# Attention and two feed-forward layers on one core: transposed tiles through four PSUM banks, and an extra copy on VectorE

## The chip, the cores and the metric

The kernel runs on one core of a Trainium2 chip. The metric is the time of one execution on the device in microseconds (us), the median over runs.

## What is computed

The reference first computes attention for 4 batches of 8 heads, 576 positions of 64 values: causal softmax attention, mixed by a gate for each head with a linear memory read.

```python
scores = scale * np.matmul(q, k.transpose(0, 1, 3, 2))
...
local = np.matmul(a, v)
...
q_p = phi(q)
mem_ret = np.einsum('bhsd,bhde->bhse', q_p, M_prev)
mem_norm = np.einsum('bhsd,bhd->bhs', q_p, z_prev)[..., None] + 1e-06
...
return (g * mem_out + (1 - g) * local).astype(np.float32)
```

The result, as 2304 tokens of 512 values, goes through two gated feed-forward layers (512 to 1536 and back, 512 to 2048 and back).

## The kernel before

**Two stages.** The attention stage takes the heads in 16 pairs (NPAIR), one pair after the other. The second stage, the two feed-forward layers, is a long run of matrix products for TensorE: up products (L1312 to L1314, from `product`) and down products. Sums that it needs of its weights and of the tokens are in part made by ScalarE, VectorE and GpSimd during the attention stage.

**A pair.** The 576 query rows of a head are one block of 64 and four blocks of 128. `tile_of(j)` gives the pair p and the tile i, and the tiles run from 4 down to 1 (tile i covers the keys up to its own block; tile 1 also has the first block of 64). For each tile TensorE computes the scores of both heads (`scores`, L1232, the first block in `scores_f`, L1242); VectorE adds the mask, negates, and takes the maxima (`tile_max`, L927); ScalarE takes the exponentials and their row sums into `rown` (`exp_tile`, L683 and L688); GpSimd puts the scaled memory rows beside them (`mem_rows`, L564), by a factor from VectorE's `mem_scale` (L946). TensorE then transposes `rown` in chunks of 128 columns (`turn`, L1261), into PSUM; a copy brings the transposed chunks into `pt` in SBUF (`copy_pt`, on ScalarE L704, on VectorE L965); and TensorE multiplies them with the values (`values`, L1287 and L1282).

**Groups and banks.** The chunks of a tile are turned in groups of two to four (GROUPS), nine groups for each pair. A group fills part of one PSUM bank, and one copy takes it out. Groups alternate between banks 4 and 5, in the order of their number n over the whole kernel, and before group n TensorE waits for the copy of group n-2. The copy of group (4, 1), the second of tile 4, is VectorE's (ON_DVE); the other eight are ScalarE's. Banks 0 to 3 hold scores. The value products go to bank 6 (tiles 4 and 3) and bank 7 (tiles 2 and 1).

**The way out.** VectorE computes the denominators and their reciprocals (`sums_inverse`, L953 and L956). TensorE transposes the reciprocals with the last group of the pair (L1265); ScalarE copies the row out (L702); SP writes it to memory in two transfers (L438, L439) and reads it back, broadcast, in two (L447). `out_x` on VectorE (L973) multiplies the value products in bank 6 (part 0) and bank 7 (part 1) with it and writes x. Each `out_x` raises `x_done`.

**TensorE's order in iteration p** is: scores of tile 4 of pair p; the last group of tile 4 and both groups of tiles 3, 2 and 1 of pair p-1, with the row-sum transpose at their end; the first-block scores of pair p; values of tile 4 of pair p-1; scores of tiles 3, 2 and 1 of pair p; the first two groups of tile 4 of pair p; values of tiles 3, 2 and 1 of pair p-1.

**VectorE's order in iteration p** is: mem_scale of tile 1 and sums_inverse of pair p-1; out_x part 0 of pair p-2; tile_max of tile 4 of pair p; out_x part 1; the norm sums (`norm_q`, `rnorm_q`); low parts for the next stage in some of the pairs (L982, L991); then mem_scale of tile 4, tile_max of tiles 3, 2 and 1, mem_scale of tile 3, the copy of group (4, 1), mem_scale of tile 2, and `phi` of the next pair (L901), from which GpSimd makes its products with z (`phi_z`, L545 and L547). All orders are written out by hand, and each engine works through its own in order.

Of the kernel before, what the change touches and what calls it, by code (L numbers as in the profile page):

```python
# [11 lines left out]
P = 128  # L12


def attention_two_ffns(nc, qk_in, nat_in, vm_in, beta, w_up, w_down, out):

    NPAIR = qk_in.shape[0]
# [6 lines left out]
    NBLK = 2 * NT - 1  # L24
# [45 lines left out]
    with ctx:  # L70
# [244 lines left out]
        def tile_of(j):  # L315

            return j // SLOTS, SLOTS - j % SLOTS
# [9 lines left out]


        GROUPS = {4: ((0, 4), (4, 8), (8, 10)), 3: ((0, 4), (4, 8)), 2: ((0, 3), (3, 6)), 1: ((0, 3), (3, 5))}
        ON_DVE = ((4, 1),)  # L330
        PER_PAIR = sum(len(g) for g in GROUPS.values())
        DVE_PER_PAIR = len(ON_DVE)
        ACT_PER_PAIR = PER_PAIR - DVE_PER_PAIR
# [1 line left out]
        def groups_before(j):  # L335

            return PER_PAIR * (j // SLOTS) + sum(len(GROUPS[SLOTS - k]) for k in range(j % SLOTS))

        def group_at(n):

            j = SLOTS * (n // PER_PAIR)
            n -= groups_before(j)
            while n >= len(GROUPS[tile_of(j)[1]]):
                n -= len(GROUPS[tile_of(j)[1]])
                j += 1
            return j, n
# [7 lines left out]
        def copied(j, g):  # L354

            d = dve_copies(j, g)
            if (tile_of(j)[1], g) in ON_DVE:
                return pt_dve, d + 1
            return pt_act, groups_before(j) + g - d + 1

        def group_bank(j, g):

            return 4 + (groups_before(j) + g) % 2

        def chunk_col(i, n):

# [24 lines left out]

        def ends_pair(j, g):

            return tile_of(j)[1] == 1 and g == 1

        def r_rows(j):

            return ps[0:NBLK, group_bank(j, 1), 2 * P:3 * P]


        def out_place(i):
# [265 lines left out]
        def _(act):  # L667
# [7 lines left out]
            def exp_tile(j):  # L675

                p, i = tile_of(j)
                w = width(i)
                at_least(act, turned, groups_before(j - ROWN + 1) if j >= ROWN else 0)
                for h in range(2):  # L680
                    t, k = 2 * j + h, block_of(i, h)
                    at_least(act, maxed, t + 1)
                    nc.scalar.activation(head_rows(j)[:, h + (i == 1), D:D + w], negs[:, t % NEGS, 0:w], ACT.Exp,  # L683
                                         bias=nmax[:, p % 2, k:k + 1], scale=-1.0,
                                         accum_out=rsum[:, p % 2, k:k + 1]).then_inc(expd, 1)
                if i == 1:
                    at_least(act, maxedf, p + 1)
                    nc.scalar.activation(head_rows(j)[:, 0, D:2 * D], negf[:, p % 2], ACT.Exp,  # L688
                                         bias=nmax[:, p % 2, 0:1], scale=-1.0,
                                         accum_out=rsum[:, p % 2, 0:1]).then_inc(expdf, 1)  # L690

            def copy_pt(j, gs):

                at_least(act, pv_done, j - PTS + 1)
                for g in range(len(GROUPS[tile_of(j)[1]])):
                    if g not in gs or (tile_of(j)[1], g) in ON_DVE:
                        continue
                    at_least(act, turned, groups_before(j) + g + 1)
                    if ends_pair(j, g):
                        p = tile_of(j)[0]  # L700
                        at_least(act, r_out, 32 * (p - 1))
                        nc.scalar.activation(rrow[0:NBLK, p % 2], r_rows(j), ACT.Copy).then_inc(r_row, 1)  # L702
                    dst, src = group_ends(j, g)
                    nc.scalar.activation(dst, src, ACT.Copy).then_inc(pt_act, 1)  # L704
# [35 lines left out]
            for p in range(NPAIR + 1):  # L740
                j = SLOTS * p
                if p > 0:
                    copy_pt(j - SLOTS, (2,))
                    for k in range(1, SLOTS):
                        copy_pt(j - SLOTS + k, (0, 1))
                if p < NPAIR:
                    exp_tile(j)
                if p + 1 < NPAIR:
                    exp_q(p + 1)
                if p < NPAIR:  # L750
                    exp_tile(j + 1)
                    copy_pt(j, (0, 1))
                    exp_tile(j + 2)
                    exp_tile(j + 3)
                for m, u, n in HIGH_AT:
                    if m == p:
                        up_high(u, n)
                for m, n in X_HIGH_AT:
                    if m == p:
                        x_high(0, n)  # L760
# [132 lines left out]
        def _(dve):  # L893
# [74 lines left out]
            def out_x(p, part):  # L968

                at_least(dve, pv_done, SLOTS * p + (2 if part == 0 else SLOTS))  # L970
                at_least(dve, r_in[p % 2], 32 * (p // 2 + 1))
                dst, o, r = x_part(p, part)
                nc.vector.tensor_tensor(dst, o, r, ALU.mult).then_inc(x_done, 1)  # L973
# [41 lines left out]
            phi(0)  # L1015
            for p in range(NPAIR + 2):
                j = SLOTS * p
                if 0 < p <= NPAIR:
                    mem_scale(j - 1)
                    sums_inverse(p - 1)  # L1020
                if p > 1:
                    out_x(p - 2, 0)
                if 0 < p < NPAIR:
                    tile_max(j)
                if p > 1:
                    out_x(p - 2, 1)
                if p < NPAIR:
                    norm_q(p)
                    dve.wait_ge(gt_set, 3)
                    rnorm_q(p)  # L1030
                for m, u, n in HIGH_AT:
                    if m == p - 1 and n > 0:
                        up_low(u, n)
                for m, n in X_HIGH_AT:
                    if m == p - 1:
                        x_low(0, n)
                if p < NPAIR:
                    mem_scale(j)
                    for k in range(1, SLOTS):
                        tile_max(j + k)  # L1040
                    mem_scale(j + 1)
                    copy_pt(j)
                    mem_scale(j + 2)
                if p + 1 < NPAIR:
                    phi(p + 1)
# [164 lines left out]
        def _(pe):  # L1210
# [34 lines left out]
            def turn(j, gs):  # L1245

                p, i = tile_of(j)
                at_least(pe, expd, 2 * (j + 1))
                at_least(pe, memd, j + 1)
                if i == 1:  # L1250
                    at_least(pe, expdf, p + 1)
                for g in range(len(GROUPS[i])):
                    if g not in gs:
                        continue
                    n = groups_before(j) + g
                    if n >= 2:
                        pe.wait_ge(*copied(*group_at(n - 2)))
                    a, b = GROUPS[i][g]
                    for c in range(a, b):
                        col = chunk_col(i, c)  # L1260
                        mm = nc.tensor.transpose(ps[:, group_bank(j, g), (c - a) * P:(c - a + 1) * P],  # L1261
                                                 rown[:, j % ROWN, col:col + P], ident[:])
                    if ends_pair(j, g):
                        pe.wait_ge(rdend, p + 1)
                        mm = nc.tensor.transpose(r_rows(j), rden[:, p % 2], ident[:])  # L1265
                    mm.then_inc(turned, 1)

            def values(j):

                p, i = tile_of(j)  # L1270
                s = p % 2
                bank, col = out_place(i)
                if i == 4:
                    at_least(pe, v_scaled, p + 1)
                    at_least(pe, x_done, 2 * p - 1)
                if i == 2:
                    at_least(pe, x_done, 2 * p)
                for g in range(len(GROUPS[i])):
                    pe.wait_ge(*copied(j, g))
                if i == 1:  # L1280
                    for h in range(2):
                        nc.tensor.matmul(ps[D * h:D * h + D, bank, 0:D], vm[:, s, h, 0], pt[:, j % PTS, 0, D * h:D * h + D],  # L1282
                                         start=True, stop=True)
                for c in range(i + 1):
                    for h in range(2):
                        n = (i + 1) * h + c + (i == 1)
                        mm = nc.tensor.matmul(ps[D * h:D * h + D, bank, col:col + P], vm[:, s, h, c],  # L1287
                                              pt[:, j % PTS, n], start=(c == 0), stop=(c == i))
                mm.then_inc(pv_done, 1)
# [147 lines left out]
```

## Time and profile before

| | |
|---|---|
| median of 3 runs | 1016.28 us (1015.73 to 1016.39) |
| the profiled execution | 1015.94 us |
| its span in the trace | 1014.1 us |
| busy, share of the span | TensorE 97%, VectorE 79%, ScalarE 57%, GpSimd 49% |
| attention stage | to about 199.7 us, when the first up product starts |

The span runs from the first to the last instruction. "Idle before" an instruction is followed by what ended it. The engines are named PE (TensorE), PEld (its weight loads), DVE (VectorE), ACT (ScalarE), POOL (GpSimd) and SP.

### The profile page before, as it was taken

What the parts mean: (1) busy time and instruction counts of PE and PEld (TensorE: products, weight loads), DVE (VectorE), ACT (ScalarE), POOL (GpSimd) and SP (SyncE); (2) the same over time, 40 slices, a digit from 0 to 9 for tenths busy, and PEclk for the clock granted to TensorE, in tenths of its full rate; (3) what the DMA queues carried; (4) which work ended last, traced back from release to release, by engine and by line L of the source; (5) the groups of instructions that cost most, each with busy time, mean ns of one, the idle gap of its engine ahead of it and who ended that gap; (6) DMA issues with size and microseconds to landing.
All of it is one profiled execution on the core that took longest, in us unless ns stands there. A gap on an engine that the chain in (4) does not pass through costs nothing.

```text
span 1014.1 us, 19135 instructions
## 1 busy us (share of the span) xinstructions
PE 982.9 (97%) x6328; PEld 919.6 (91%) x6328; DVE 799.9 (79%) x1422; ACT 573.1 (57%) x1130; POOL 501.5 (49%) x407
## 2 busy tenths in 40 slices
PE   6999999999999999999999999999999999999998
PEld 4777777788999999999999998999989999899997
DVE  5778888556788776778767789888897888988776
ACT  5898898755445544446444445545554546555451
POOL 5666766256675432454333476575543435432330
PEclk9999999999999999999999999999999999999999
DMA  6454443134334333233333323324132522225211
GB/s 228 145 155 161 155 143 118 50 125 146 104 111 144 114 112 104 104 106 125 105 104 107 124 82 104 116 72 146 63 125 65 185 101 87 97 91 187 68 37 63
DMA packets 34782, 116.13 MB, mean 115 GB/s; under 512 B 4224, under 2 KB 4608, under 8 KB 34688
## 3 DMA queue, kind: packets, MB, share of 16 engines
q1 hardware_dynamic: 34544, 114.91, 33.9%
q8 instruction: 55, 0.90, 0.4%
q14 instruction: 39, 0.32, 0.1%
q10 hardware_dynamic: 144, 0.00, 0.0%
HBM read 100.14 MB, written 14.75 MB: 113 GB/s over the span
## 4 chain that ended last, share of the span: by engine, by line
PE 85%; DVE 5%; issue 4%; ACT 4%; POOL 1%; DMA 1%; DVEq 0%; ACTq 0%; POOLq 0%
PE ps L1312 24%; PE ps L1313 23%; PE ps L1314 23%; PE ps L1261 5%; PE ps L1287 5%; PE ps L1232 5%; ACT pt L704 2%; DVE xt_l L991 1%; DVE xy L1106 1%; DVE hid_l L1084 1%; DVE hid_r L1096 1%; ACT rown L683 1%; DMA qk<-qk_in 0%; ACT tmp L806 0%; DVE hb L1061 0%
## 5 line engine op out<-in xcount | busy, mean ns | idle before, releaser
L589 POOL TENSOR_TENSOR wu_l<-wu_r,wu_h 128x768 fp32r<-128x768 f32 (+1 forms) x75 | 142.1, 1902 | 399.0 <-ACT wu_h L713 399.0
L1312 PE MATMUL ps<-xt_h,wu_h 128*128 128x384 f32 x840 | 283.2, 337 | 5.5 <-DVE xt_l L991 2.8
L1314 PE MATMUL ps<-xt_h,wu_l 128*128 128x384 f32 x840 | 280.9, 334 | 0.0
L1313 PE MATMUL ps<-xt_l,wu_h 128*128 128x384 f32 x840 | 280.9, 334 | 0.0
L1312 PE MATMUL ps<-hid_h,wd_h 128*128 128x384 f32 x672 | 226.4, 337 | 6.3 <-DVE xy L1106 5.6
L1314 PE MATMUL ps<-hid_h,wd_l 128*128 128x384 f32 x672 | 224.7, 334 | 0.0
L1313 PE MATMUL ps<-hid_l,wd_h 128*128 128x384 f32 x672 | 224.7, 334 | 0.0
L1106 DVE TENSOR_TENSOR xy<-xy,ps 128x384 f32<-128x384 f32 x288 | 157.1, 548 | 48.4 <-PE ps L1314 47.4
L791 ACT ACTIVATE hid_h<-hid_r 128x768 fp32r<-128x768 f32 x84 | 70.8, 842 | 198.7 <-DVE hid_r L1080 141.9
L1312 PEld LDWEIGHTS ps<-xt_h,wu_h 128*128 128x128 f32 x840 | 157.6, 188 | 13.7 <-issue 11.8
L1313 PEld LDWEIGHTS ps<-xt_l,wu_h 128*128 128x128 f32 x840 | 157.7, 188 | 0.0
L1314 PEld LDWEIGHTS ps<-xt_h,wu_l 128*128 128x128 f32 x840 | 157.7, 188 | 0.0
L595 POOL TENSOR_TENSOR wd_l<-wd_r,wd_h 128x512 fp32r<-128x512 f32 x84 | 136.1, 1633 | 15.0 <-ACT wd_h L718 13.9
L1312 PEld LDWEIGHTS ps<-hid_h,wd_h 128*128 128x128 f32 x672 | 126.1, 188 | 12.4 <-issue 8.0
L982 DVE TENSOR_TENSOR wu_l<-wu_r,wu_h 128x512 fp32r<-128x512 f32 x105 | 123.8, 1179 | 8.0 <-DMA kept<-wu_r 3.9
L1313 PEld LDWEIGHTS ps<-hid_l,wd_h 128*128 128x128 f32 x672 | 126.2, 188 | 0.0
L1314 PEld LDWEIGHTS ps<-hid_h,wd_l 128*128 128x128 f32 x672 | 126.1, 188 | 0.0
L713 ACT ACTIVATE wu_h<-wu_r 128x512 fp32r<-128x512 f32 (+1 forms) x180 | 118.9, 694 | 0.0
L1084 DVE TENSOR_TENSOR hid_l<-hid_r,hid_h 128x768 fp32r<-128x768 f32 x84 | 85.8, 1022 | 36.9 <-ACT hid_h L791 36.8
L683 ACT ACTIVATE rown<-negs,nmax 128x576 f32<-128x576 f32 (+3 forms) x128 | 77.0, 603 | 12.3 <-DVE nmax L927 12.3
L1261 PE MATMUL ps<-ident,rown 128*128 128x128 f32 x464 | 74.2, 286 | 7.8 <-ACT pt L704 2.5
L1261 PEld LDWEIGHTS ps<-ident,rown 128*128 128x128 f32 x464 | 49.4, 142 | 30.0 <-ACT pt L704 16.1
(84 smaller groups left out, 1319.3 us busy)
## 6 DMA issues: line engine op xcount, KB each, us to landing
wu_r<-w_up SPq DMA_DIRECT2D x60, 512.0 KB, 4.7
wd_r<-w_down SPq DMA_DIRECT2D x42, 512.0 KB, 3.7
wu_r<-kept SPq DMA_DIRECT2D x38, 512.0 KB, 5.5
kept<-wu_r SPq DMA_DIRECT2D x19, 512.0 KB, 4.5
qk<-qk_in SPq DMA_DIRECT2D x15, 640.0 KB, 5.1
nat<-nat_in SPq DMA_DIRECT2D x16, 384.0 KB, 3.1
vm<-vm_in SPq DMA_DIRECT2D x16, 320.0 KB, 3.6
rbc<-rsums SPq DMA_DIRECT2D x32, 144.0 KB, 3.1
```

The costliest lines, as they stand in the source:

```text
L589: nc.gpsimd.tensor_tensor(wu_l[u % 3][:, a:b], wu_r[u % 3][:, a:b], wu_h[u % 2][:, a - 1:b - 1].bitcast(F32), ALU.subtract).then_inc(low_p ...
L595: nc.gpsimd.tensor_tensor(wd_l[:, t % 6], wd_r[:, t % 6], wd_h[:, t % 6].bitcast(F32), ALU.subtract).then_inc(wd_lo, 1)
L683: nc.scalar.activation(head_rows(j)[:, h + (i == 1), D:D + w], negs[:, t % NEGS, 0:w], ACT.Exp, bias=nmax[:, p % 2, k:k + 1], scale=-1.0, ...
L713: nc.scalar.activation(wu_h[u % 2][:, a - 1:b - 1], wu_r[u % 3][:, a:b], ACT.Copy).then_inc(wu_hi[n], 1)
L791: nc.scalar.activation(hid_h[:, t % 6], hid_r[:, t % 6], ACT.Copy).then_inc(hh_done, 1)
L982: nc.vector.tensor_tensor(wu_l[u % 3][:, a:b], wu_r[u % 3][:, a:b], wu_h[u % 2][:, a - 1:b - 1].bitcast(F32), ALU.subtract).then_inc(low_d ...
L1084: nc.vector.tensor_tensor(hid_l[:, t % 6], hid_r[:, t % 6], hid_h[:, t % 6].bitcast(F32), ALU.subtract).then_inc(hl_done, 1)
L1106: nc.vector.tensor_tensor(y, y, o, ALU.add).then_inc(evac, 1)
L1261: mm = nc.tensor.transpose(ps[:, group_bank(j, g), (c - a) * P:(c - a + 1) * P], rown[:, j % ROWN, col:col + P], ident[:])
L1312: nc.tensor.matmul(dst, w_hi, v_hi, start=start, stop=False, skip_group_check=onto)
L1313: nc.tensor.matmul(dst, w_hi, v_lo, start=False, stop=False, skip_group_check=onto)
L1314: return nc.tensor.matmul(dst, w_lo, v_hi, start=False, stop=stop, skip_group_check=onto)
```

## The change

Each group gets a fixed bank from a table, among four banks: (4,0), (4,2), (2,1) and (1,1) use bank 4; (4,1), (3,0) and (1,0) bank 5; (3,1) bank 6; (2,0) bank 7. `group_under` finds the group that used the same bank last, and the turn waits for its copy. Before a turn into bank 6 or 7 TensorE also waits for the x multiplication of that bank of the pair before, and the values of tile 4 wait for the copy of (3,1). The row-sum transpose moves from the last group of the pair to the one before it. On VectorE both out_x move to the head of the iteration, and a copy, that of group (2,0), is added behind tile_max of tile 4. On ScalarE the exponentials of tile 2 move ahead of the copy of (4,0).

```diff
--- before.py
+++ after.py
@@ -327,7 +327,11 @@
 
         GROUPS = {4: ((0, 4), (4, 8), (8, 10)), 3: ((0, 4), (4, 8)), 2: ((0, 3), (3, 6)), 1: ((0, 3), (3, 5))}
-        ON_DVE = ((4, 1),)
+        ON_DVE = ((4, 1), (2, 0))
+
+
+
+        BANK = {(4, 0): 4, (4, 1): 5, (4, 2): 4, (3, 0): 5, (3, 1): 6, (2, 0): 7, (2, 1): 4, (1, 0): 5, (1, 1): 4}
         PER_PAIR = sum(len(g) for g in GROUPS.values())
         DVE_PER_PAIR = len(ON_DVE)
         ACT_PER_PAIR = PER_PAIR - DVE_PER_PAIR
@@ -360,7 +364,15 @@
 
         def group_bank(j, g):
 
-            return 4 + (groups_before(j) + g) % 2
+            return BANK[tile_of(j)[1], g]
+
+
+        def group_under(j, g):
+
+            n = groups_before(j) + g - 1
+            while n >= 0 and group_bank(*group_at(n)) != group_bank(j, g):
+                n -= 1
+            return group_at(n) if n >= 0 else None
 
         def chunk_col(i, n):
 
@@ -391,11 +403,11 @@
 
         def ends_pair(j, g):
 
-            return tile_of(j)[1] == 1 and g == 1
+            return tile_of(j)[1] == 1 and g == 0
 
         def r_rows(j):
 
-            return ps[0:NBLK, group_bank(j, 1), 2 * P:3 * P]
+            return ps[0:NBLK, group_bank(j, 0), 3 * P:4 * P]
 
         def out_place(i):
@@ -749,8 +761,8 @@
                     exp_q(p + 1)
                 if p < NPAIR:
                     exp_tile(j + 1)
+                    exp_tile(j + 2)
                     copy_pt(j, (0, 1))
-                    exp_tile(j + 2)
                     exp_tile(j + 3)
                 for m, u, n in HIGH_AT:
                     if m == p:
@@ -1015,15 +1027,16 @@
             phi(0)
             for p in range(NPAIR + 2):
                 j = SLOTS * p
+                if p > 1:
+                    out_x(p - 2, 0)
+                    out_x(p - 2, 1)
                 if 0 < p <= NPAIR:
                     mem_scale(j - 1)
                     sums_inverse(p - 1)
-                if p > 1:
-                    out_x(p - 2, 0)
                 if 0 < p < NPAIR:
                     tile_max(j)
-                if p > 1:
-                    out_x(p - 2, 1)
+                if 0 < p <= NPAIR:
+                    copy_pt(j - 2)
                 if p < NPAIR:
                     norm_q(p)
                     dve.wait_ge(gt_set, 3)
@@ -1252,9 +1265,10 @@
                 for g in range(len(GROUPS[i])):
                     if g not in gs:
                         continue
-                    n = groups_before(j) + g
-                    if n >= 2:
-                        pe.wait_ge(*copied(*group_at(n - 2)))
+                    if group_under(j, g):
+                        pe.wait_ge(*copied(*group_under(j, g)))
+                    if group_bank(j, g) >= 6:
+                        at_least(pe, x_done, 2 * (p - 1) + group_bank(j, g) - 5)
                     a, b = GROUPS[i][g]
                     for c in range(a, b):
                         col = chunk_col(i, c)
@@ -1273,6 +1287,7 @@
                 if i == 4:
                     at_least(pe, v_scaled, p + 1)
                     at_least(pe, x_done, 2 * p - 1)
+                    pe.wait_ge(*copied(j + 1, 1))
                 if i == 2:
                     at_least(pe, x_done, 2 * p)
                 for g in range(len(GROUPS[i])):
```

## Rows read from the trace of the kernel before

**Rows 1.** Busy time of each engine over the span, from the page.

```profile
PE 982.9 (97%) x6328; PEld 919.6 (91%) x6328; DVE 799.9 (79%) x1422; ACT 573.1 (57%) x1130; POOL 501.5 (49%) x407
```

**Rows 2.** Row-sum transposes: count, duration min/median/max in ns, first and last start.

```profile
L1265 PE MATMUL ps<-ident,rden x16: 272/273/273, 21.4 to 196.1; 128*9 128x128 f32 x16
```

**Rows 3.** Stretches: length; PE, PEld, DVE, ACT, POOL busy (count); granted clock, DMA, GB/s.

```profile
145.00:156.63 11.63, 11.27 (x114) 8.30 (x115) 9.92 (x33) 10.55 (x31) 7.99 (x10) 1.00 0.48 150
199.60:211.20 11.60, 11.60 (x70) 11.54 (x67) 4.41 (x10) 5.59 (x9) 0.00 (x0) 1.00 0.47 129
```

**Rows 4.** Timeline of TensorE's weight loads: start, length, count, idle before.

```profile
87.94 0.64 PEld L1261 LDWEIGHTS ps<-ident,rown 128*128 128x128 f32 x6
88.92 0.42 PEld L1261 LDWEIGHTS ps<-ident,rown 128*128 128x128 f32 x4 [0.34 <-ACT pt L704]
...
90.88 0.31 PEld L1261 LDWEIGHTS ps<-ident,rown 128*128 128x128 f32 x3 [0.31 <-issue]
91.39 0.20 PEld L1261 LDWEIGHTS ps<-ident,rown 128*128 128x128 f32 x2 [0.20 <-ACT pt L704]
...
91.67 0.30 PEld L1242 LDWEIGHTS ps<-qk 128*128 128x128 f32 x2
...
95.10 0.86 PEld L1261 LDWEIGHTS ps<-ident,rown 128*128 128x128 f32 x8 [0.23 <-issue]
```

**Rows 5.** Timeline of ScalarE in the same pair.

```profile
88.48 0.38 ACT L704 ACTIVATE pt<-ps 128x256 f32<-128x256 f32 x1
88.92 0.60 ACT L704 ACTIVATE pt<-ps 128x512 f32<-128x512 f32 x1
...
90.27 0.49 ACT L704 ACTIVATE pt<-ps 128x384 f32<-128x384 f32 x1
...
91.98 0.27 ACT L702 ACTIVATE rrow<-ps 9x128 f32<-9x128 f32 x1
92.15 0.36 ACT L704 ACTIVATE pt<-ps 128x256 f32<-128x256 f32 x1
92.41 0.76 ACT L683 ACTIVATE rown<-negs,nmax 128x576 f32<-128x576 f32 x1
...
95.08 0.67 ACT L683 ACTIVATE rown<-negs,nmax 128x448 f32<-128x448 f32 x1 [0.48 <-DVE nmax L927]
```

**Rows 6.** Timeline of VectorE in the same pair.

```profile
87.73 0.16 DVE L946 SCALAR_TENSOR_TENSOR mscale<-rsum,rnorm 128x3 f32<-128x3 f32 x1 [0.40 <-ACT rown L688]
...
89.30 0.37 DVE L973 TENSOR_TENSOR xy<-ps,rbc 128x256 f32<-128x256 f32 x1
89.59 0.75 DVE L927 CUSTOM_DVE_ANT_0 negs<-ps,mask 128x576 f32<-128x576 f32 x1
...
90.94 0.49 DVE L973 TENSOR_TENSOR xy<-ps,rbc 128x320 f32<-128x320 f32 x1
...
97.04 0.68 DVE L965 COPY pt<-ps 128x512 f32<-128x512 f32 x1
98.09 0.16 DVE L946 SCALAR_TENSOR_TENSOR mscale<-rsum,rnorm 128x2 f32<-128x2 f32 x1 [0.37 <-ACT rown L683]
```

**Rows 7.** Timeline of SP's transfers in the same pair.

```profile
92.99 0.62 SPq L439 DMA_DIRECT2D rsums<-rrow  x1
94.77 1.13 SPq L447 DMA_DIRECT2D rbc<-rsums  x2
```

**Rows 8.** The 32 reads of the row sums, L447.

```profile
DMA to landing us min/median/max: 2.8/3.1/4.6
```

**Rows 9.** Timeline of GpSimd in the same pair.

```profile
87.83 1.27 POOL L547 TENSOR_TENSOR qz<-qp,nat 128x512 f32<-128x512 f32 x1
...
94.36 0.40 POOL L564 TENSOR_TENSOR rown<-qp,mscale 128x128 f32<-128x128 f32 x1 [1.97 <-DVE mscale L946]
```

**Rows 10.** The 16 denominators, L953: durations in ns.

```profile
L953 DVE TENSOR_SCALAR den<-rsum x16: 172/1292/1297, 18.6 to 192.5; 128x9 f32<-128x9 f32 x16
```

**Rows 11.** VectorE's copies from PSUM in the later stage, L1103.

```profile
L1103 DVE COPY xy<-ps x48: 543/552/559, 238.0 to 916.1; 128x384 f32<-128x384 f32 x48
```

## The prediction, made before the changed kernel ran

> **What bounds the kernel now.** The page first: TensorE is busy 97% of the span [rows 1], at the full granted clock in the stretches looked at [rows 3]. So only time in which TensorE stands still, or its instruction count, can move the end. The change touches nothing behind the attention stage, so the second view is that stage's own beat. The transpose of the reciprocal row sums comes once for each of the 16 pairs, first at 21.4 us and last at 196.1 us [rows 2]: 174.7 / 15 = 11.65 us for each pair. The up products behind the stage leave TensorE no pause (11.60 of 11.60 us busy), so what the stage gives back reaches the end; within a pair ScalarE is busy 10.55 of 11.63 us and VectorE 9.92 [rows 3].
>
> The third view is TensorE's weight loads in one pair, because every transpose begins with one and the idle time stands before it. The section with the last group of tile 4 and all of tiles 3, 2 and 1 begins at 87.94 and ends with the load for the first-block scores at 91.67: 3.73 us for 21 transposes and that of the row sums. Eight transposes without a pause take 0.86 us, 0.108 each, so 22 would take 2.38. The missing 1.35 us is in five gaps of 0.20 to 0.34, one ahead of each group from the third on (three of them shown) [rows 4]. ScalarE's copies show why: with two banks, group n waits for the copy of group n-2. Tile 4's last copy ends at 88.48 + 0.38 = 88.86 and the next group starts at 88.92; the copy of (2,0) ends at 90.76 and (1,0) starts at 90.88 [rows 4, 5]. Outside this section TensorE has no pause in the pair that waits for another engine. So the loop is: turn, copy, turn, five times, and then TensorE's own work.
>
> **What the four banks take away.** Group (3,1) goes to bank 6 and (2,0) to bank 7, where their last users are the two x products. Then the first five groups need only the copies of (4,2), done at 88.86, and (3,0). Run through from 87.94 at 0.108: (3,0) at 88.22, (3,1) at 88.66, (2,0) at 89.09, (2,1) at 89.42 (bank 4, free since 88.86), (1,0) at 89.75 (bank 5, freed by the copy of (3,0) at 88.92 + 0.60 = 89.52). The row-sum transpose follows at 90.07; it is only moved, at no cost in itself. (1,1) could start at 90.18, but shares bank 4 with (2,1).
>
> ScalarE by then: back to back, a copy starts 0.09 before the one before it ends (91.98 with 0.27 is followed at 92.15, that with 0.36 at 92.41) [rows 5]. (3,0) 88.92 to 89.52, (3,1) 89.43 to 90.03; (2,0) is VectorE's now; (2,1) 89.94 to 90.43. TensorE follows 0.05 later, at 90.48. So one wait of 0.30 us is left of five. Before, (1,1) started at 91.39 and the first-block scores 0.28 behind it; the row-sum transpose, 0.11 of that, is now in front, so 0.17 is left: 90.48 + 0.17 = 90.65 against 91.67. **Gain 1.02 us for each section.**
>
> **What the added wait costs.** (3,1) and (2,0) now wait for the two x multiplications of the pair before, and behind them in TensorE's queue stands everything. They used to start at 89.30 and 90.94 [rows 6]; at those places they would stop TensorE for 0.3 and then nearly 2 us. They are moved to the head of VectorE's order, behind phi, where VectorE was idle 0.40 us before 87.73. At 0.29 and 0.40 start to start they end near 88.1: ahead of 88.66 and 89.09. The values they read were all produced by 86.8. They also need the broadcast row sums: the second write is issued at 92.99, the reads from 94.77 on, in 1.13 for the two [rows 7], and a read landed in 3.1 in the median and 4.6 at worst [rows 8]. One period back the second of them is there at 86.8, in the median, against 87.33, where phi ends. The row is copied 1.5 us earlier in the new order (ScalarE reaches it at 90.4, not 91.98), in a period that is 1.0 shorter: the slack grows by 0.5. I take nothing for this wait. SP's reads of the row sums, and what waits for x before the sums of the next stage, get x earlier than before; the order of SP and GpSimd is not touched. The value product of tile 4, in bank 6 too, now waits for the copy of (3,1), which ends at 90.03, before the product's turn.
>
> **What is queued behind the moved work.** The mem_scale of tile 1 goes from 87.73 [rows 6] to about 88.1. GpSimd, its reader, comes to it only at 89.1, after the product with z that starts at 87.83 and takes 1.27 [rows 9]: covered. If GpSimd were ahead, (1,0) would be late by up to 0.4, of which 0.30 is under the remaining copy wait. The denominator is stretched anyway: 1.29 us in the median, 0.17 at the least, in the last section, where GpSimd had no such product to do [rows 10]; here it ends with GpSimd's product. So a later start leaves its end, and the maxima of the next tile 4 start at 89.30 in place of 89.59; at 1.35 for both [rows 6] their last result is there at 90.73, just as the first-block scores need it. Here the margin is about nothing.
>
> The Trainium skill, SBUF — State Buffer, section "SBUF: two separate sides", says the pair of ports that VectorE and GpSimd share is an exclusive lock, held for a whole instruction; the two lengths of the denominator agree. It speaks against the change in one point: mem_scale has two SBUF inputs and would now fall inside GpSimd's product and be held to its end (rival 1). By it the sum would be 1.02 - 0.29 a section; by the rows alone, 1.02.
>
> **The extra copy on VectorE.** The trace has no 128x384 copy to pt on VectorE; the same shape from PSUM takes 0.55 in the later stage [rows 11], between a bound of 0.68 (the 128x512 copy at 97.04) [rows 6] and nothing if it falls into idle time. I take 0.55, 0.47 start to start. It stands behind the maxima, so at 90.65 to 91.2; its reader, the value product of tile 2, runs more than 3 us later. On VectorE it delays the norm sums, but those start at 91.12 and not 91.34, as two x multiplications have left. ScalarE loses 0.40 start to start: before (1,1), and so tile 4's exponentials start at 91.3 and not 92.41. What hangs on them is GpSimd's memory rows, which ended at 94.36 + 0.40 = 94.76 [rows 9]; now 1.1 earlier, 93.7, for the next turn of tile 4 at 95.10 - 1.02 = 94.08 [rows 4]: covered by 0.4.
>
> **Two exponentials ahead of tile 4's first copy.** ScalarE idles 0.48 before the exponentials of tile 3 at 95.08 [rows 5], and tile 2's maxima are there by the time it ends these. The copy moves back by two 128x320 exponentials, 1.09 us; it then ends near 97.0, and its bank is next written at the following section's start, at 98.5. Nothing on either side.
>
> **Sum.** 16 sections: 16 x 1.02 = 16.3 us. The profiled execution took 1015.94, 0.34 below the median of 1016.28; the difference is taken from the median: **1000.0**. Bounds: with no wait left, 16 x 1.35 = 21.6, 994.7.
>
> **Rivals.**
> 1. VectorE late for the first-block scores. mem_scale is held until 89.1, the denominator comes after it, the maxima end 0.29 later: 16 x 0.73 = 11.7, 1004.6. For it: the margin of nothing. Against: tile 2's exponentials now come before the copy, so phi and GpSimd's product start earlier in the pair by some 0.4. 14%.
> 2. VectorE becomes the bound. 9.92 busy in a pair with a low part of x [rows 3], plus 0.47, plus its short pauses and the 0.37 it waited for tile 2's exponentials before 98.09 [rows 6]: 11.1 at worst, 16 x 0.53 = 8.5, 1007.8. Against: 1.1 of the 9.92 is the denominator's waiting, which shrinks as the queue gets later. 12%.
> 3. Slower: the row sums' round trip becomes a loop. Row-sum transpose, copy (0.36), two writes (0.75), 1.78 until the reads, 0.53, landing 3.1 to 3.4, x multiplications 0.8, (2,0) to the row-sum transpose 1.3: 8.9 us in the median, 10.4 with a landing of 4.6. It decides from 11.6 on, that is 2.7 us more in the two transfers than in the median. At 12.0 it gives +16 x 0.4 = +6.4, 1022.7. 8%. Between 10.6 and 11.6 it eats the gain.
> 4. The change does not show: the next stage waits for the last x anyway, or the loop of 3 stands at today's beat: 1016. Against: no pause in the 11.6 us of up products, with the last x product inside them [rows 3]. 6%.
> 5. The last wait vanishes too: 994.7. 6%.
>
> **Chances.** The forecast, 998 to 1002, 54%; rivals 14, 12, 8, 6, 6. A measurement of this kernel tells 0.2%, 2 us. Faster 54 + 14 + 12 + 6 = 86%, same 6%, slower 8%. The range takes the forecast, rivals 1 and 2 and the edge of 5: 995 to 1008.5; alone, the forecast has 998 to 1002.
>
> **What would show it.** Row-sum transposes 10.6 us apart; in each section one idle gap of the weight loads, 0.3 us, ahead of the last group, and none before (3,1) or (2,0); the x multiplications ending before 88.66 of this pair's clock; denominator stretched to GpSimd's end still; VectorE with a 128x384 copy of 0.55. Wrong if a gap before (3,1) is ended by VectorE's x product or by the row-sum DMA (rival 3), if one stands before the first-block scores, ended by the maxima (rival 1), or if ScalarE's exponentials of tile 4 come late for its turn.

## The result, and the profile after

The changed kernel takes 1000.34 us in the median of four runs (999.02 to 1001.57), the kernel before 1016.17 in four (1015.73 to 1016.39). The ratio is 0.9845, with a 95% interval of 0.9827 to 0.9862: 15.8 us less. The forecast was 1000.0. The profiled execution took 999.02, the lowest of the four; its span is 997.2. Below, "stage" is the time up to the first up product of the profiled execution: 199.66 before, 184.86 after, 14.80 less.

From the page after, the busy time of each engine over the span:

```profile
PE 970.6 (97%) x6328; PEld 920.4 (92%) x6328; DVE 795.7 (80%) x1438; ACT 562.7 (56%) x1114; POOL 503.8 (51%) x407
```

The 16 copies have gone from ScalarE (1130 to 1114) to VectorE (1422 to 1438); TensorE has the same 6328 instructions in 16.9 us less span. VectorE's busy time does not rise with the 16 copies (8.8 us): summed over the trace its mem_scales take 8.4 us more and its denominators 17.0 us less. The 4.2 us by which it falls lie in other groups, mostly low parts for the second stage (L982, now L994, 2.4 less), and no run was made for them. Here are these groups. First the row-sum transposes, then the denominators and the mem_scales (count, duration in ns, first and last start):

```profile
L1279 PE MATMUL ps<-ident,rden x16: 272/273/273, 20.7 to 180.8; 128*9 128x128 f32 x16
...
L965 DVE TENSOR_SCALAR den<-rsum x16: 157/159/174, 19.5 to 179.0; 128x9 f32<-128x9 f32 x16
...
L958 DVE SCALAR_TENSOR_TENSOR mscale<-rsum,rnorm x64: 150/158/962, 13.6 to 178.9; 128x2 f32<-128x2 f32 x48, 128x3 f32<-128x3 f32 x16
```

The beat is (180.8 - 20.7) / 15 = 10.67 us against 11.65 [rows 2]. No denominator is stretched any more, where 1292 ns was the median [rows 10]; mem_scales of up to 962 ns have come instead. One pair in the middle, with a low part of x (columns as in [rows 3]):

```profile
133.80:144.49 10.69, 10.49 (x118) 8.33 (x113) 9.88 (x34) 9.85 (x29) 7.96 (x9) 1.00 0.51 158
```

TensorE has the full clock here too. VectorE and ScalarE are both within 0.85 us of the beat now. Next one pair's weight loads, as in [rows 4]:

```profile
82.75 2.05 PEld L1275 LDWEIGHTS ps<-ident,rown 128*128 128x128 f32 x19
84.77 0.09 PEld L1279 LDWEIGHTS ps<-ident,rden 128*9 128x9 f32 x1
85.35 0.20 PEld L1275 LDWEIGHTS ps<-ident,rown 128*128 128x128 f32 x2 [0.49 <-ACT pt L716]
85.52 0.30 PEld L1255 LDWEIGHTS ps<-qk 128*128 128x128 f32 x2
85.89 1.07 PEld L1302 LDWEIGHTS ps<-pt,vm 128*64 128x64 f32 x20
```

The turning section (the last group of tile 4 and all groups of tiles 3, 2 and 1, up to the load for the first-block scores) runs from 82.75 to 85.52, 2.77 us against 3.73, with 19 transposes in one piece and one gap, ahead of (1,1). The view counts 0.49 from the end of the last load; from the row-sum load (84.77) to the next is 0.58 where 0.11 is the pace, so some 0.47 is lost there. ScalarE and VectorE in the same pair:

```profile
83.28 0.39 ACT L716 ACTIVATE pt<-ps 128x256 f32<-128x256 f32 x1
...
83.72 1.09 ACT L716 ACTIVATE pt<-ps 128x512 f32<-128x512 f32 x2
...
84.81 0.49 ACT L716 ACTIVATE pt<-ps 128x384 f32<-128x384 f32 x1
```

```profile
81.57 0.81 DVE L985 TENSOR_TENSOR xy<-ps,rbc 128x256 f32<-128x256 f32 x2
82.53 0.93 DVE L958 SCALAR_TENSOR_TENSOR mscale<-rsum,rnorm 128x3 f32<-128x3 f32 x1
83.38 0.16 DVE L965 TENSOR_SCALAR den<-rsum 128x9 f32<-128x9 f32 x1
...
84.37 0.75 DVE L939 CUSTOM_DVE_ANT_0 negs<-ps,mask 128x576 f32<-128x576 f32 x1
...
85.05 0.55 DVE L977 COPY pt<-ps 128x384 f32<-128x384 f32 x1
```

The x multiplications end at 82.38, before the section begins, so (3,1) and (2,0) never wait for them. The maxima end at 85.12, 2.37 after the section's start. GpSimd beside it:

```profile
82.15 1.28 POOL L559 TENSOR_TENSOR qz<-qp,nat 128x512 f32<-128x512 f32 x1
```

mem_scale, 0.15 to 0.16 at the other tiles, is 0.93 long and ends at 83.46, with GpSimd's product (82.15 + 1.28 = 83.43). So it is in the other pairs: in this execution 14 of the 16 mem_scales of tile 1 start inside the product, take 0.20 to 0.96, and every one of them ends 0.02 to 0.03 behind it. The Trainium skill, SBUF — State Buffer, section "SBUF: two separate sides", has the ports that VectorE and GpSimd share as an exclusive lock, held for the whole instruction. The trace agrees: each mem_scale ends when the product does, whenever it started.

In the waits between 20 and 170 us (total us, times, longest), the two that decide between the forecast and rival 3:

```profile
PEld ps L1275 <- ACT pt L716: 6.4, 13, 0.5
...
DVE xy L985 <- DMA rbc<-rsums: 3.5, 5, 1.1
```

By the weight loads the one gap, 0.47 us, stands in every pair from the second to the fifteenth (13 of them in this window); VectorE waits for the row sums 5 times, 1.1 us at most, and TensorE never for x.

### The profile page after: what moved, and what is told of

The parts are those of the page before. It is cut to its first block, busy times and chain, and to the rows that moved or that the text cites. A ratio compares the mean times of both kernels' runs of the same rounds, so it can differ in the third digit from the quotient of the medians.

```text
span 997.2 us, 19181 instructions
## 1 busy us (share of the span) xinstructions
PE 970.6 (97%) x6328; PEld 920.4 (92%) x6328; DVE 795.7 (80%) x1438; ACT 562.7 (56%) x1114; POOL 503.8 (51%) x407
## 4 chain that ended last, share of the span: by engine, by line
PE 83%; DVE 6%; ACT 5%; issue 4%; DMA 1%; POOL 1%; SPq 0%; DVEq 0%; ACTq 0%; POOLq 0%
PE ps L1327 24%; PE ps L1329 23%; PE ps L1328 23%; PE ps L1302 5%; PE ps L1245 4%; ACT pt L716 3%; PE ps L1275 3%; DVE xt_l L1003 1%; DVE xy L1119 1%; DVE hid_l L1097 1%; DVE hid_r L1109 1%; ACT rown L695 1%; DMA qk<-qk_in 1%; DMA rbc<-rsums 0%; DVE negs L939 0%
## 5 line engine op out<-in xcount | busy, mean ns | idle before, releaser
L994 DVE TENSOR_TENSOR wu_l<-wu_r,wu_h 128x512 fp32r<-128x512 f32 x105 | 121.4, 1156 | 6.9 <-DMA kept<-wu_r 3.9
L818 ACT ACTIVATE tmp<-hb,nhalf 128x768 f32<-128x768 f32 x48 | 45.1, 940 | 50.8 <-issue 45.9
L1103 DVE SCALAR_TENSOR_TENSOR tmp<-tmp 128x768 f32<-128x768 f32 x48 | 54.9, 1144 | 19.3 <-ACT tmp L818 18.7
```

The source lines that it names most:

```text
L994: nc.vector.tensor_tensor(wu_l[u % 3][:, a:b], wu_r[u % 3][:, a:b], wu_h[u % 2][:, a - 1:b - 1].bitcast(F32), ALU.subtract).then_inc(low_d ...
L1103: nc.vector.scalar_tensor_tensor(tmp[:, r], tmp[:, r], 1.0, tmp[:, r], ALU.min, ALU.mult).then_inc(s_done, 1)
```

## The experiments

All are edits of the changed kernel. The beat is worked out from the first and last row-sum transpose, as above.

| kernel | median us | ratio to before, 95% | beat us | stage us |
|---|---|---|---|---|
| changed | 1000.34 | 0.9827 to 0.9862 | 10.67 | 184.86 |
| e5 two banks | 1014.62 | 0.9976 to 0.9995 | 11.53 | 198.16 |
| e1 copy on ScalarE | 1003.65 | 0.9866 to 0.9895 | 10.93 | 188.96 |
| e6 copy twice | 1000.60 | 0.9832 to 0.9861 | 10.67 | 184.58 |
| e2 copy before exponentials | 1002.61 | 0.9856 to 0.9885 | 10.86 | 187.70 |
| e3 row sums last | 1002.31 | 0.9849 to 0.9878 | 10.82 | 186.78 |
| e4 x late | 1034.32 | 1.0160 to 1.0194 | 12.98 | 220.5 |
| e7 last group later | 1001.92 | 0.9847 to 0.9877 | 10.83 | 187.01 |
| e8 GpSimd's order | 1025.07 | 1.0077 to 1.0111 | 12.33 | 208.9 |
| e9 with SP's order | 1000.38 | 0.9829 to 0.9856 | 10.71 | 184.46 |
| e10 last group in bank 6 | 998.24 | 0.9809 to 0.9836 | 10.62 | 183.54 |
| e11 e10 and e9 | 997.64 | 0.9806 to 0.9833 | 10.58 | 182.54 |

**The banks.** e5 keeps every order of the change, but takes two banks in turn and leaves the copy of (2,0) to ScalarE.

```
-            return BANK[tile_of(j)[1], g]
+            return 4 + (groups_before(j) + g) % 2
```

> All orders of the changed kernel (x first, row sums with the last group but one, tile 2's exponentials ahead of the copy), but banks 4 and 5 in turn as before, and all copies but (4,1) on ScalarE. Theory (the banks and the shorter chain of copies bring the gain): the gaps ahead of (3,1), (2,0), (2,1), (1,0) and (1,1) are all back, the beat is 11.5 to 11.65 us, 1013.5 to 1016.5 us. Rival (the orders bring it): 1000 to 1005.

1014.62, as expected: of the 15.8 us the orders alone give 1.3 (by the ratio, 0.5 to 2.4). So nearly all of the gain needs the banks. e1, next, differs from e5 only in the banks and their waits, and takes 1003.65: the banks give 11.0 us, and the copy's move to VectorE, on top of them, 3.3.

**The copy on VectorE.** e1 puts (2,0) back on ScalarE; e6 makes VectorE's copy of (2,0) twice, the second behind the first's end.

```
-        ON_DVE = ((4, 1), (2, 0))
+        ON_DVE = ((4, 1),)
```

> The changed kernel with the copy of group (2,0) back on ScalarE; banks, order and the rest as changed. Theory (the one wait left in a turning section stands on ScalarE's chain of copies up to that of (2,1)): the chain gets one 128x384 copy longer, 0.40 to 0.49 us, so the idle gap ahead of (1,1) grows from 0.37 to about 0.8 and the beat from 10.69 to about 11.1 us; 15 sections give +6 to +7, 1006 to 1008 us. Rival (the copy only balances work, the banks do it all): 1000 to 1001.

1003.65, 2.4 to 4.4 us less than expected. The weight loads show where, and why not more:

```profile
84.18 2.05 PEld L1275 LDWEIGHTS ps<-ident,rown 128*128 128x128 f32 x19
...
87.06 0.20 PEld L1275 LDWEIGHTS ps<-ident,rown 128*128 128x128 f32 x2 [0.76 <-ACT pt L716]
```

The gap ahead of (1,1) is 0.76, not 0.49: one more copy ahead of (2,1)'s costs 0.27 a section. In this pair it takes 0.37 start to start (86.13 to 86.50), and 0.10 of that falls into time in which ScalarE had been waiting for the turn of (2,1).

```
+                        if i == 2:
+                            nc.vector.tensor_copy(dst, src).then_inc(pt_more, 1)
+                            dve.wait_ge(pt_more, tile_of(j)[0] + 1)
                         nc.vector.tensor_copy(dst, src).then_inc(pt_dve, 1)
```

> The changed kernel with VectorE's copy of group (2,0) made twice, the second behind a wait for the first. Theory (VectorE has room behind the maxima of tile 4: it idles 0.97 us before mem_scale of tile 4): nothing, 999.5 to 1001.5 us, the idle time shrinks by about 0.6. Rival (VectorE is the bound or near it): +0.6 us a pair, 1006 to 1009.

1000.60 and an unchanged beat, as expected: VectorE has room for a second 0.55 us behind the maxima. It isn't the bound (rival 2).

**The exponentials first.** e2 puts tile 4's first copies back between the exponentials.

```
-                    exp_tile(j + 2)
                     copy_pt(j, (0, 1))
+                    exp_tile(j + 2)
```

> The changed kernel with ScalarE's order of before: the copy of (4,0) ahead of the exponentials of tile 2. Theory: bank 4 is due only in the next section, and the other side has slack too, so nothing or up to +0.1 us a section: 1000.3 to 1002 us, with mem_scale of tile 2, phi and GpSimd's product 0.4 us later in the beat. Rival (the maxima of tile 4 then come too late for the first-block scores): +0.3 us a section, 1004 to 1006.

1002.61; the beat is 0.19 longer, more than expected, though less than the rival's price. VectorE's order and TensorE's weight loads in one pair, one view after the other:

```profile
83.85 1.14 DVE L958 SCALAR_TENSOR_TENSOR mscale<-rsum,rnorm 128x3 f32<-128x3 f32 x1
84.92 0.16 DVE L965 TENSOR_SCALAR den<-rsum 128x9 f32<-128x9 f32 x1
...
85.91 0.75 DVE L939 CUSTOM_DVE_ANT_0 negs<-ps,mask 128x576 f32<-128x576 f32 x1
```

```profile
83.81 1.73 PEld L1275 LDWEIGHTS ps<-ident,rown 128*128 128x128 f32 x16
85.71 0.31 PEld L1275 LDWEIGHTS ps<-ident,rown 128*128 128x128 f32 x3 [0.17 <-issue]
...
86.42 0.20 PEld L1275 LDWEIGHTS ps<-ident,rown 128*128 128x128 f32 x2 [0.34 <-ACT pt L716]
86.79 0.30 PEld L1255 LDWEIGHTS ps<-qk 128*128 128x128 f32 x2 [0.17 <-issue]
```

Without the move, phi and GpSimd's product come later in the pair. mem_scale is held for 1.14, tile 1's memory rows are late for (1,0) (GpSimd ends them at 85.65; gap of 0.17), and the maxima end at 86.66, 2.85 after the section's start and not 2.37, so that the first-block scores wait as well. That is rival 1's mechanism; the swap on ScalarE is what keeps it off.

**The row sums' place.** e3 puts their transpose back behind (1,1).

```
-            return tile_of(j)[1] == 1 and g == 0
+            return tile_of(j)[1] == 1 and g == 1
```

> The changed kernel with the row-sum transpose back at the last group, (1,1). Theory: the transpose, 0.11 us, no longer lies in front of the copy wait but behind it, and the row of sums leaves about 0.5 us later, which the slack of its round trip takes: +0.11 us a section, 1001 to 1003 us, beat 10.8, and VectorE's idle time before the x multiplications, ended by the row-sum transfer, grows by about 0.4 us a pair. Rival (the round trip is already the loop that sets the beat): +0.5 us a section, 1007 or more.

1002.31, beat 0.15 longer, stage 1.92 longer. The transpose and its load fill 0.11 of the wait when they stand ahead of (1,1); that is 16 x 0.11 = 1.8. The other half of the expectation did not come: VectorE's idle time ended by the row-sum transfer is 3.0 us in 4 times between 20 and 170 us, not longer than the 3.5 of the changed kernel.

**x late.** e4 keeps the banks, but leaves the x multiplications where they were on VectorE.

```
+                if p > 1:
+                    out_x(p - 2, 0)
                 if 0 < p < NPAIR:
                     tile_max(j)
+                if p > 1:
+                    out_x(p - 2, 1)
```

> The changed kernel with the two x multiplications at their old places in VectorE's order, part 0 ahead of and part 1 behind the maxima of tile 4. Theory (the wait for x is free only because x leaves first): (3,1) waits for part 0, about 0.6 us, and (2,0) for part 1, until the maxima are done, so a section gets about 2.1 us longer than with the change: a beat of about 12.8 us, slower than the kernel before, 1028 to 1035 us. Rival (the row sums' round trip or the port lock sets the place of x anyway): under 1005.

1034.32, slower than before. In its waits between 20 and 170 us:

```profile
PE ps L1276 <- DVE xy L985: 18.2, 21, 1.1
```

Two of the four banks are x's; without x first TensorE waits for x 21 times, and the change costs 18 us instead of giving 16.

**Where the last wait can go.** e7 turns (1,1) after the values of tile 4, and copies it behind the exponentials of tile 4.

```
-                        copy_pt(j - SLOTS + k, (0, 1))
+                        copy_pt(j - SLOTS + k, (0, 1) if k < SLOTS - 1 else (0,))
...
-                        turn(SLOTS * (p - 1) + k, (0, 1))
+                        turn(SLOTS * (p - 1) + k, (0, 1) if k < SLOTS - 1 else (0,))
...
+                    turn(SLOTS * (p - 1) + SLOTS - 1, (1,))
```

> The changed kernel with the turn of the last group, (1,1), moved behind the values of tile 4 on TensorE, and its copy behind the exponentials of tile 4 on ScalarE. Theory (the wait ahead of (1,1), 0.37 us and 0.06 of restart, is the one left): it goes, but the first-block scores now wait for the maxima of tile 4, which end 2.38 us after the section's start against 2.24 for TensorE: about -0.23 us a section, beat 10.45, 996 to 998 us. Rival (GpSimd's scaling of the values, done 2.57 us after the section's start, or the exponentials of tile 4 take the wait's place): 1000 or more.

1001.92: a miss, and of the wrong sign.

```profile
105.45 2.06 PEld L1277 LDWEIGHTS ps<-ident,rown 128*128 128x128 f32 x19
...
107.95 0.30 PEld L1257 LDWEIGHTS ps<-qk 128*128 128x128 f32 x2 [0.38 <-issue]
108.35 1.10 PEld L1304 LDWEIGHTS ps<-pt,vm 128*64 128x64 f32 x20
109.63 0.20 PEld L1277 LDWEIGHTS ps<-ident,rown 128*128 128x128 f32 x2 [0.17 <-issue]
```

```profile
107.07 0.75 DVE L941 CUSTOM_DVE_ANT_0 negs<-ps,mask 128x576 f32<-128x576 f32 x1
```

The gap went to the first-block scores, 0.38, which now wait for the maxima (the last ends at 107.82, in the second view); they start at 2.50 after the section's start and not at 2.77. The 0.27 saved is what the two moved transposes take, and they come again behind, 0.20 long and with 0.17 of idle time on their way in. The expectation has no term for these 0.37.

e10 leaves the order and puts (1,1) in bank 6 instead, with the value products of tiles 4 and 3 in bank 7.

```
-        BANK = {(4, 0): 4, ..., (1, 0): 5, (1, 1): 4}
+        BANK = {(4, 0): 4, ..., (1, 0): 5, (1, 1): 6}
-            return (6, P * (i - 3)) if i >= 3 else (7, D + P * (i - 1))
+            return (7, P * (i - 3)) if i >= 3 else (6, D + P * (i - 1))
```

> The changed kernel with the last group, (1,1), in bank 6 in place of bank 4, and the value products of tiles 4 and 3 in bank 7, those of tiles 2 and 1 in bank 6; values of tile 4 wait for the copy of (2,0) in place of that of (3,1). Theory (the one wait left in a section is that of (1,1) for the copy of (2,1)): bank 6 is free 2.06 us after the section's start, TensorE comes at 2.24, so the gap of 0.49 goes; the first-block scores then follow the maxima, 2.44, and the values of tile 4 the copy of (2,0) at 2.85 to 2.9 in place of 3.14: beat 10.42 to 10.5, 996 to 997.5 us. Rival (VectorE's maxima and its copy take the whole wait over): 999.5 or more.

998.24: lower by 2.1 in the medians and 1.3 in the stage, less than expected. The intervals of the two kernels overlap, their runs do not (997.73 to 998.83 against 999.02 to 1001.57).

```profile
93.33 2.06 PEld L1275 LDWEIGHTS ps<-ident,rown 128*128 128x128 f32 x19
...
95.47 0.25 PEld L1275 LDWEIGHTS ps<-ident,rown 128*128 128x128 f32 x2
95.83 0.30 PEld L1255 LDWEIGHTS ps<-qk 128*128 128x128 f32 x2
96.36 1.10 PEld L1303 LDWEIGHTS ps<-pt,vm 128*64 128x64 f32 x20 [0.23 <-issue]
```

The wait ahead of (1,1) is gone. But the values of tile 4 start at 3.03 after the section's start, where the changed kernel has 3.14: they write bank 7 now and wait for VectorE's copy of (2,0), which stands behind the maxima and ends at 96.18 (95.63 + 0.55).

**What holds mem_scale.** e8 lets GpSimd make the product with z after tile 1's memory rows and the scaling of the values; e9 also moves SP's load for it behind the reads of the row sums. In e9:

```
-                if p + 2 < NPAIR:
-                    load_nat(p + 2)
                 if p > 1:
...
                 read_r(p - 1)
+                if p + 2 < NPAIR:
+                    load_nat(p + 2)
...
                     v_scale(p - 1)
+                    if p < NPAIR:
+                        phi_z(p)
```

> The changed kernel with GpSimd's products with z behind its memory rows of tile 1 and its scaling of the values, in place of ahead of them. Theory (mem_scale of tile 1 is held 0.93 us only because GpSimd's product is under way, and nothing but the first section pays for it): mem_scale back to 0.16 and the denominator at 0.16, the maxima of tile 4 earlier by about 0.7 us, the beat unchanged at 10.69, the first turning section shorter by about 0.8 us: 999 to 1000 us. Rival (the long mem_scale is not a held port but its own cost at that place): it stays at 0.9 and the time at 1000.3 or more.

1025.07, slower than before by 0.8 to 1.1%, where 999 to 1000 was expected: a miss, and of the wrong sign. mem_scale and denominator take 0.15 and 0.16, as expected (one mem_scale of tile 1 takes 0.39, inside GpSimd's memory rows), so it is what GpSimd does at the time that stretches them, and not their place on VectorE. The waits from 30 to 200 us and SP's transfers in one pair show what I had left out:

```profile
DVE xy L985 <- DMA rbc<-rsums: 29.7, 13, 3.7
```

```profile
110.09 0.33 SPq L439 DMA_DIRECT2D nat<-nat_in  x1
...
110.95 0.68 SPq L450 DMA_DIRECT2D rsums<-rrow  x1
...
114.30 1.12 SPq L459 DMA_DIRECT2D rbc<-rsums  x2
```

load_nat waits for the product (it overwrites its input), and the row sums' writes and reads stand behind it in SP's queue. Later product, later row sums, later x, and with x in front of everything on VectorE the banks come late (TensorE waits for x 11 times, 11.6 us together, in the same stretch): the loop of rival 3, with a beat of 12.33. It decides once something delays the row sums.

> The order of GpSimd of the run before (products with z behind the memory rows and the value scaling), and on SP the load of q rows for the pair after next moved behind the writes and reads of the row sums. Theory (the run before was slow because that load waits for the products with z, and the row sums queue behind it on SP): the row sums leave in time again, mem_scale takes 0.16, the maxima of tile 4 end 0.7 us earlier, the beat is that of the changed kernel, 10.69, as TensorE's turn of (2,1) and its copy set it; only the first section gains, 0.8 us: 998.5 to 1000.5 us. Rival (moving GpSimd's products costs by itself, through the norm sums and tile 4's memory rows): over 1003.

1000.38: with the load out of the way the 25 us are back, and the time is that of the changed kernel. So the held mem_scale costs nothing in the steady beat (10.71 by the table, 10.69 from section to section in most pairs of both kernels). It does in the first pair, whose rows are these: VectorE's and GpSimd's in the changed kernel, TensorE's there, TensorE's in e9.

```profile
18.65 0.96 DVE L958 SCALAR_TENSOR_TENSOR mscale<-rsum,rnorm 128x3 f32<-128x3 f32 x1 [0.83 <-ACT rown L695]
```

```profile
18.32 1.27 POOL L559 TENSOR_TENSOR qz<-qp,nat 128x512 f32<-128x512 f32 x1
```

```profile
17.78 1.74 PEld L1275 LDWEIGHTS ps<-ident,rown 128*128 128x128 f32 x16
20.27 0.31 PEld L1275 LDWEIGHTS ps<-ident,rown 128*128 128x128 f32 x3 [0.75 <-issue]
...
21.41 0.30 PEld L1255 LDWEIGHTS ps<-qk 128*128 128x128 f32 x2 [0.50 <-issue]
```

```profile
17.58 2.06 PEld L1275 LDWEIGHTS ps<-ident,rown 128*128 128x128 f32 x19
...
20.45 0.30 PEld L1255 LDWEIGHTS ps<-qk 128*128 128x128 f32 x2
```

There the first section takes 3.63 (17.78 to 21.41) in the changed kernel and 2.87 in e9. Of these 0.76 us the stage keeps 0.40 (184.46 against 184.86), and the medians show none.

**Both.** e11 is e10 with e9's edits.

> The two runs before together. Theory (without the last copy wait the section is held by VectorE's maxima and copy, which are late only because mem_scale of tile 1 is held by GpSimd's product): both waits go, TensorE runs through the section, beat 10.3 to 10.4, 994.5 to 996.5 us. Rival (the row sums' round trip, or tile 4's exponentials, now sets the beat): 997 or more.

997.64, the lowest of all, though not apart from e10 by the intervals. 994.5 to 996.5 was expected; the rival, that tile 4's exponentials or the row sums now set the beat, had 997 or more. In the pair below the section has no gap left; the next turn of tile 4 has one instead, 0.47 where the changed kernel has 0.23, right behind GpSimd's memory rows of tile 4 (97.57 + 0.40 = 97.97, second view):

```profile
92.01 2.06 PEld L1275 LDWEIGHTS ps<-ident,rown 128*128 128x128 f32 x19
...
94.36 0.30 PEld L1255 LDWEIGHTS ps<-qk 128*128 128x128 f32 x2
...
98.04 0.86 PEld L1275 LDWEIGHTS ps<-ident,rown 128*128 128x128 f32 x8 [0.47 <-issue]
```

```profile
97.57 0.40 POOL L576 TENSOR_TENSOR rown<-qp,mscale 128x128 f32<-128x128 f32 x1 [0.51 <-DVE mscale L958]
```

The product with z comes later, VectorE's norm sums wait for it (17.2 us in 15 times between 20 and 170), and tile 4's mem_scale and memory rows, which need the norms, are late. So it is neither of the rival's two, but the norms that come late.

## Why the prediction was right, and which terms were off

The time was right by the mechanism forecast: e5 and e1 show that the banks give it, e4 that it hangs on x first. That it was right to 0.3 us is luck: the stage gave 1.5 us less than the sum, about 1.0 came from where the sum had nothing, and the reason given for one term did not hold. The terms in turn:

- **Gain 1.02 us for each section.** 0.96 in the pair shown, and 11.65 - 10.67 = 0.98 of the mean beat. The forecast had the load of (1,1) 2.54 after the section's start; it came at 2.60. The gap is 0.47 and not 0.30, as TensorE also came to it 0.11 sooner than forecast (2.13, not 2.24), which costs nothing. The copy of (2,1) starts at 2.06, not 2.00: (3,0) and (3,1) were copied on time, but the copy of (2,1) could not start before its own turn was over, at 84.71. I had run ScalarE's chain back to back and not laid it against the turn.
- **Sum.** 16 sections were to give 16.3; the stage gave 14.80. The sum took one pair's section for all 16. By the weight loads of every pair, the thirteen sections like it went from 3.72 to 2.77, 0.07 short of the forecast each. The second (4.03 to 2.77) and the last (4.92 to 3.68) gave more, 1.26 and 1.24. The first gave only 0.33. These rows bound it in the kernel before:

```profile
17.60 0.64 PEld L1261 LDWEIGHTS ps<-ident,rown 128*128 128x128 f32 x6
...
21.56 0.30 PEld L1242 LDWEIGHTS ps<-qk 128*128 128x128 f32 x2
```

That is 3.96 against 3.63 after, with (1,0) waiting for memory rows behind a mem_scale held for 0.96: rival 1's mechanism, in the one place where nothing comes early enough, and e9 takes 0.76 of it away. All 16 sections together gave 15.2, and 0.4 of that was lost again outside them. So the 1.5 us missing are 0.9 (thirteen sections) and 0.7 (the first), less 0.5 (second and last), plus 0.4.

- **The rest of the 15.8.** By the medians 1.0 comes from outside the stage, where I took nothing; by the two profiled executions 2.1 (16.9 of span, 14.80 of stage). The part behind the stage takes 814.4 us before and 812.3 after, and 812.3 to 815.1 in the profiled executions of all thirteen kernels, which run the same second stage. No experiment was made for this; it stays open whether it is more than that spread.
- **What the added wait costs: nothing.** Right. x ended at 82.38, 0.37 before the section. The slack was real but rests on SP's order too, which I had looked at only as "not touched"; e8 and e9 show that this order, once GpSimd's product comes later, is worth 25 us.
- **mem_scale of tile 1: covered.** Right in its price, wrong in its reason. The rows alone had it short and early; it was held to the end of GpSimd's product, as rival 1 and the Trainium skill's lock in the section named above had it, and the denominator lost its stretch in return (0.16). The price is nothing while the maxima end at 2.37: the first-block scores are then still waiting their turn behind (1,1), until 2.77. The margin is 0.4, not "about nothing". e7, which takes (1,1) away, uses it up.
- **The extra copy on VectorE.** 0.55, the length taken from [rows 11]. Rival 2 falls with e6: a second copy costs nothing. What it takes off ScalarE is worth 0.27 a section (e1).
- **Two exponentials ahead: "Nothing on either side".** This step was wrong. The swap is worth 0.19 a pair, 2.3 us by the medians (e2), because it brings phi and GpSimd's product forward. I had named just this as the argument against rival 1, and still priced the edit at nothing.
- **Row-sum transpose moved, "at no cost in itself".** Right; that it then fills 0.11 of the wait, as the sum had it, is confirmed by e3.
- **Rival 3.** It didn't come here, but e8 made it real: a delay of the row sums in SP's queue set a beat of 12.33. That this is near the 12.0 that it was priced with is chance; the price was for longer transfers, not for a queue.
- **Rival 5.** With the last wait gone (e10) the time is 998.24, not 994.7: the next waits, VectorE's copy of (2,0) and then tile 4's memory rows (e11), stand close behind.

## What to carry to other kernels

When a ring of buffers is widened with banks that another tenant also uses, the gain is the gaps less one new order: price first what releases the borrowed banks (here x, back through the broadcast, the row sums and every transfer queued ahead of them), since being late there costs more than the banks give. Lay each engine's chain against the others step by step, with the later of "free" and "ready" at each. A swap that costs its own engine nothing can still move what hangs behind it: follow it to the reader of the reader.

## What was not expected of the hardware

A mem_scale of 128x3 elements with both inputs in SBUF took 0.93 and 1.14 us in the pairs shown when it started inside a GpSimd 128x512 tensor_tensor, and ended 0.03 behind that product's end in the first; the profile counts this as busy, not as idle with a releaser, so that no wait points to GpSimd. Moved out of the product (e8, e9) the same instruction takes 0.15 to 0.16, but for one of 0.39 in each of these runs. In the kernel before it was the denominator, with one input, that was stretched in the same way [rows 10].

Not every GpSimd instruction does it. The scaling of the norms, also with two inputs in SBUF, starts in 15 of the 16 pairs of the changed kernel inside a GpSimd tensor_scalar of 128x576 elements (L549, 1.65 us), and is never longer than 0.172:

```profile
L924 DVE SCALAR_TENSOR_TENSOR norms<-norm,gt x16: 169/170/172, 13.1 to 172.0; 128x9 f32<-128x9 f32 x16
```

No run was made on what sets the two apart.
